# Attention and two MLPs on one core: another order and split of the work for the first tile of tokens

## The chip, the cores and the metric

The kernel runs on one core of one Trainium2 chip. The metric is the device time of one execution in microseconds (us). A core has TensorE for matmuls (PE in the rows; PEld is its weight load), VectorE (DVE), ScalarE (ACT), GpSimd (POOL) and SyncE (SP, here only a queue that issues transfers). SPq and POOLq are the queues' own issuing time.

## The reference, cut to what matters

Chunked attention with 8 batches, 8 heads, 576 tokens and 64 numbers a head, then two feed-forward layers, all in float32.

```
scores = scale * q_c @ k_c.T            # inside chunks of 64 tokens
attn   = exp(scores - max(scores)) ; attn = attn / (sum(attn) + 1e-9)
x      = attn @ v_c                     # 4608 tokens x 512
x      = relu(x @ w_in_a)**2 @ w_out_a  # 512 -> 2048 -> 512
h      = x @ w_in_b
out    = where(h >= 1, h, where(h <= -1, 0, (h + 1)**2 / 4)) @ w_out_b
```

## The kernel before

The 4608 tokens are cut into 9 tiles of 512, a tile into 4 groups of 128 tokens (two chunks, 8 heads). Float32 products of the two MLPs are made of three rounded ones: each matrix is split into a high and a low part, so x, the hidden values and the weights each need a "hi" cast (ScalarE) and a "lo" subtraction (VectorE, or GpSimd for weights).

While the MLP of tile t runs, the attention of tile t+1 is spread over its 16 slices. Each slice has 12 matmuls `up` (L350) and 12 `down` (L385 in the first MLP, L389 in the second). The first tile has no such cover: its four groups run ahead of everything, on a path of their own, and this is the part that the change touches. For group g:

- SyncE loads q and k (`load_qk`, L182, four transfers of 128 KB) and v (`load_v`, L191, two).
- TensorE turns q, then k, by matmuls with the identity (`turn`, L403, 8 matmuls) into two banks of `acc`. VectorE copies them out (`copy_qk`, L669 and twice L673: q, and k's even and odd heads apart, between zeros).
- TensorE makes the scores (`score`, L418, 16 matmuls), for odd groups in a bank of `h_ps`, so that two groups' scores can stand at once.
- VectorE finds each head's maximum and the bias (`find_max`, L679, L683). ScalarE makes the exponentials head by head, 8 instructions that also sum (`exponentials`, L535). VectorE adds 1e-9 and inverts (`invert`, L689, L691), GpSimd multiplies (`normalise`, L281).
- TensorE turns the probabilities (`turn_probs`, L431, 32 matmuls), ScalarE copies them to a block diagonal (`copy_turned`, L547), TensorE multiplies v by it (`head_out`, L449, 16 matmuls). The result is split into x hi (L552, once L779 on VectorE) and x lo (L645).

Then come the first MLP slices f = 0 and 1 of tile 0 in two halves of 256 tokens (`up_half`, L363): the first halves need groups 0 and 1, the second ones all four. Slices 2 to 15 run whole. Group 4 is the first of tile 1; its scores stand between `up_half` and slice 0's `down`, and its q and k are turned by TensorE as well. From group 5 on VectorE turns q and k by 16 block transposes (L660) and the probabilities by 8 (L709), in a fixed order among its `hid_lo` subtractions (L736).

GpSimd loads the weights slice by slice (`load_in` L257, `load_out` L264, 256 KB each) into two places each; ScalarE casts them (L514, L520), GpSimd subtracts (L270, L275). A third load of a kind waits for the first one's subtraction.

Every engine runs its list in the order written; between engines there are only counting semaphores. So the order of the lists, which the change rewrites for the first tile, decides who waits.

## Time and profile before

| | us |
|---|---|
| median of 3 runs | 1685.73 (1684.38 to 1686.45) |
| the profiled execution, its own time | 1684.03 |
| its span | 1682.2 |
| TensorE busy | 1659.6 |
| VectorE, ScalarE, GpSimd busy | 870.6, 623.7, 130.7 |

The span runs from the first to the last instruction of the trace. The profiled execution took 1.8 us more than its span, and 1.7 us less than the median. "Idle before" in a row is time in which the engine had nothing running, with the instruction that ended it behind an arrow. Where the profile holds no clock record yet, at the start, it prints a granted clock of 1.00.

### The profile page before, as it was taken

The page shows a single profiled execution, that of the slowest core. Times are in us where ns is not written, and L with a number is a line of the kernel's source. Part 1 is how long each engine was busy: PE and PEld are TensorE (multiplying, and loading weights), DVE is VectorE, ACT ScalarE, POOL GpSimd, SP SyncE. Part 2 cuts the span into 40 slices and gives each one's busy share as a digit, 9 for nine tenths or more (in the row PEclk, how much of TensorE's full clock was granted, in tenths as well). Part 3 has the DMA queues.
Part 4 walks back from the last instruction along what each step waited for, and adds up shares of the span by engine and source line. Part 5 has one row for each costly group of instructions (what it writes and reads, how often), then busy time and mean ns, then how long its engine had stood idle before and what let it go on. Part 6 is the DMA issues. An engine that isn't in the chain of part 4 may idle for free.

```text
span 1682.2 us, 22443 instructions
## 1 busy us (share of the span) xinstructions
PE 1659.6 (99%) x8256; PEld 1369.8 (81%) x8256; DVE 870.6 (52%) x1630; ACT 623.7 (37%) x1476; POOL 130.7 (8%) x139
## 2 busy tenths in 40 slices
PE   6999999999999999999999999999999999999999
PEld 5788888888888888888888888888888888888887
DVE  4776666666666676674113444443444444344433
ACT  4664444444444444443553222222222222222222
POOL 3650000000000000000472000000000000000000
PEclk9999999999999999999999999999999999999999
DMA  7442111121212121120331010101010101010000
GB/s 157 119 107 64 38 48 35 52 49 26 58 38 63 27 56 39 26 63 26 108 98 70 1 51 1 51 1 52 1 50 1 51 1 50 1 34 17 16 10 26
DMA packets 126670, 74.93 MB, mean 45 GB/s; under 512 B 115552, under 2 KB 115552, under 8 KB 124256
## 3 DMA queue, kind: packets, MB, share of 16 engines
q1 hardware_dynamic: 121440, 56.64, 12.5%
q0 software_dynamic: 5120, 16.78, 3.3%
q8 instruction: 74, 1.21, 0.3%
q14 instruction: 36, 0.29, 0.1%
HBM read 54.53 MB, written 18.87 MB: 44 GB/s over the span
## 4 chain that ended last, share of the span: by engine, by line
PE 97%; DVE 1%; DMA 1%; SPq 0%; issue 0%; ACT 0%
PE h_ps L350 46%; PE acc L385 24%; PE acc L389 23%; PE heads_out_ps L449 2%; PE scores_ps L418 2%; DMA qk_in<-in_k_dram 1%; SPq L182 0%; PE acc L403 0%; PE h_ps L363 0%; DVE q_t_and_k_t_by_head L660 0%; PE acc L431 0%; PE acc L449 0%; DVE hidden_split L736 0%; DVE v_and_probs_diag L709 0%; DVE x_t_split L645 0%
## 5 line engine op out<-in xcount | busy, mean ns | idle before, releaser
L350 PE MATMUL h_ps<-x_t_split,w_in_split 128*128 128x512 f32 x3432 | 825.3, 389 | 1.1 <-issue 1.1
L350 PEld LDWEIGHTS h_ps<-x_t_split,w_in_split 128*128 128x128 f32 x3432 | 644.2, 188 | 136.3 <-issue 3.1
L385 PE MATMUL acc<-hidden_split,w_out_split 128*128 128x512 f32 x1728 | 419.5, 392 | 3.3 <-DVE hidden_split L736 3.3
L389 PE MATMUL acc<-w_out_split,hidden_split 128*128 128x512 f32 x1728 | 415.2, 389 | 0.9 <-DVE hidden_split L736 0.9
L385 PEld LDWEIGHTS acc<-hidden_split,w_out_split 128*128 128x128 f32 x1728 | 321.9, 188 | 74.8 <-issue 9.3
L389 PEld LDWEIGHTS acc<-w_out_split,hidden_split 128*128 128x128 f32 x1728 | 324.2, 188 | 68.5 <-ACT hidden_split L571 1.3
L736 DVE TENSOR_TENSOR hidden_split<-hidden_raw,hidden_split 128x512 fp32r<-128x512 f32 x288 | 199.8, 694 | 317.4 <-ACT hidden_split L571 317.3
L731 DVE SCALAR_TENSOR_TENSOR hidden_raw<-hidden_raw 128x512 f32<-128x512 f32 x144 | 99.7, 692 | 353.0 <-ACT hidden_raw L566 353.0
L571 ACT CAST hidden_split<-hidden_raw 128x512 fp32r<-128x512 f32 x288 | 178.7, 621 | 218.2 <-DVE hidden_raw L734 213.6
L561 ACT ACTIVATE hidden_raw<-h_ps 128x512 f32<-128x512 f32 x144 | 86.1, 598 | 424.6 <-PE h_ps L350 423.1
L566 ACT ACTIVATE hidden_raw<-h_ps 128x512 f32<-128x512 f32 x144 | 86.1, 598 | 369.0 <-PE h_ps L350 369.0
L660 DVE STREAM_TRANSPOSE q_t_and_k_t_by_head<-qk_in 32x256 f32<-32x256 f32 x496 | 216.1, 436 | 8.0
L709 DVE STREAM_TRANSPOSE v_and_probs_diag<-probs 32x256 f32<-32x256 f32 x256 | 111.6, 436 | 3.5
L734 DVE TENSOR_TENSOR hidden_raw<-h_ps,hidden_raw 128x512 f32<-128x512 f32 x144 | 99.5, 691 | 4.9
L563 ACT ACTIVATE hidden_raw<-hidden_raw 128x512 f32<-128x512 f32 x144 | 91.0, 632 | 4.6
L535 ACT ACTIVATE probs<-scores_ps,exp_bias 128x64 f32<-128x64 f32 x272 | 81.0, 324 | 26.0 <-DVE exp_bias L683 26.0
L679 DVE TENSOR_REDUCE score_max<-scores_ps 128x8 f32<-128x512 f32 x34 | 23.5, 691 | 90.0 <-PE scores_ps L418 89.9
L257 POOL DMA_DIRECT2D qk_in<-in_moe_w_in_dram x16 | 12.2, 765 | 655.0 <-DVE q_t_and_k_t_by_head L660 650.8
L535 ACT ACTIVATION_READ_ACCUMULATOR probs<-scores_ps,exp_bias 128x1 f32 x272 | 58.9, 217 | 0.0
L418 PE MATMUL scores_ps<-q_t_and_k_t_by_head 128*64 128x128 f32 x544 | 36.5, 278 | 2.3 <-DVE q_t_and_k_t_by_head L673 2.3
L449 PEld LDWEIGHTS heads_out_ps<-v_and_probs_diag 128*64 128x64 f32 x544 | 29.0, 136 | 11.5 <-issue 11.3
L449 PE MATMUL heads_out_ps<-v_and_probs_diag 128*64 128x128 f32 x544 | 37.2, 279 | 0.0
(60 smaller groups left out, 444.6 us busy)
## 6 DMA issues: line engine op xcount, KB each, us to landing
qk_in<-in_q_dram SPq DMA_DIRECT2D x72, 128.0 KB, 3.0
qk_in<-in_k_dram SPq DMA_DIRECT2D x72, 128.0 KB, 3.1
v_and_probs_diag<-in_v_dram SPq DMA_DIRECT2D x72, 128.0 KB, 3.0
mlp_out_t<-stage SPq DMA_DIRECT2D x9, 1024.0 KB, 4.3
v_and_probs_diag<-mlp_out_t SPq DMA_DIRECT2D x9, 1024.0 KB, 7.0
out_dram<-stage SPq DMA_DIRECT2D x8, 1024.0 KB, 5.0
stage<-in_moe_w_in_dram POOLq DMA_DIRECT2D x16, 256.0 KB, 3.3
stage<-in_moe_w_out_dram POOLq DMA_DIRECT2D x16, 256.0 KB, 3.5
```

Of the source, the lines that this page charges most:

```text
L350: last = nc.tensor.matmul(h_ps[:, bank, :], w_in[:, kt, w, cols], x_t[:, par, x, kt, :], start=(kt == 0 and w == HI and x == HI), stop=(kt ...
L385: last = nc.tensor.matmul(acc[:, j, :], w_out[:, f, w, cols], hid[:, half, x, :], start=first, stop=end)
L389: last = nc.tensor.matmul(acc[:, j, :], hid[:, half, w, cols], w_out[:, f, x, :], start=first, stop=end)
L449: last = nc.tensor.matmul(out_ps_of(n)[rows, head // 2, :], v_in[:, par, head * D:(head + 1) * D], probs_diag_of(n)[:, head, :], start=Tru ...
L535: last = nc.scalar.activation(probs_of(n)[:, pair, keys], s_ps_of(n)[:, pair, keys], ACT.Exp, scale=SCALE, bias=bias[:, par, head:head + 1 ...
L563: nc.scalar.activation(raw[:, half, :], raw[:, half, :], ACT.Square).then_inc(raw_ready, 1)
L571: nc.scalar.copy(hid[:, half, HI, :], raw[:, half, :]).then_inc(hid_hi, 1)
L660: last = nc.vector.transpose(dst, src)
L709: last = nc.vector.transpose(probs_diag[at:at + BLK, :, tok * BLK:(tok + 1) * BLK], heads[tok * BLK:(tok + 1) * BLK, :, wid * BLK:(wid + 1 ...
L731: nc.vector.scalar_tensor_tensor(out=a, in0=a, scalar=1.0, in1=a, op0=ALU.min, op1=ALU.mult).then_inc(squared, 1)
L734: nc.vector.tensor_tensor(a, h_ps[:, half, :], a, ALU.max).then_inc(raw_ready, 1)
L736: nc.vector.tensor_tensor(hid[:, half, LO, :], a, hid[:, half, HI, :].bitcast(F32), ALU.subtract).then_inc(hid_lo, 1)
```

## The change

It rewrites the first tile's path and what goes with it:

- TensorE runs 10 identity matmuls (128x128) into `out_ps` as soon as the identity stands, ahead of the first `turn`.
- k of groups 0 and 1 is loaded from ScalarE's queue (4 transfers), q of both from SyncE's. q and k of group 2 are issued ahead of v of group 0.
- The copies after `turn` are split: ScalarE copies q and k's odd heads, VectorE k's even heads. Group 4's are all made on VectorE.
- Softmax of groups 0 to 3: VectorE takes the maximum, subtracts it for the whole row (PSUM to SBUF), ScalarE makes one exponential of 128x512 in place of 8 of 128x64, VectorE sums by a reduction of its own. Group 3 is normalised on VectorE.
- The scores of all groups stand in one bank; `score(n)` waits until the group before has been shifted.
- GpSimd's first weight load stands behind its first `normalise`, and its order after that is new. ScalarE casts the first input weights after the fourth exponential, the second ones after x hi of group 2 and the turned copy of group 3. TensorE's order at the end of the path is new: `turn(4)` moves behind head_out(1) and turn_probs(2).
- In slice f = 1 of tile 0 VectorE makes `hid_lo` first and normalises and turns group 4 after it.

```diff
@@ SyncE, GpSimd
                     for which, blocks in ((0, q_blocks), (1, k_blocks)):
+                        if which == 1 and not past(g, 2):
+                            continue
...
+            load_qk(2, 0)
             load_v(0, 0)
-            load_qk(2, 0)
...
-            pool.wait_ge(k_turned, 1)
+            normalise(0, 0)
             load_in(0, 0, stage)
-            normalise(0, 0)
+            normalise(1, 1)
             load_in(1, 0, stage)
+            normalise(2, 0)
+            load_out(0, 0, stage)
             weights_in(0, 0, stage)
-            normalise(1, 1)
-            load_out(0, 0, stage)
             load_in(2, 0, stage)
-            normalise(2, 0)
             load_out(1, 0, stage)
             weights_in(1, 0, stage)
-            normalise(3, 1)
@@ TensorE
-                if f == 1:
-                    pe.wait_ge(exped, GROUPS)
...
-                elif n >= 2:
-                    pe.wait_ge(exped, n - 1)
+                elif n > 0:
+                    pe.wait_ge(shifted, n)
...
+            for i in range(WARM):
+                nc.tensor.matmul(out_ps[:, i % HP, :], ident[:], ident[:], start=True, stop=True)
             turn(0)
             for g in range(GROUPS):
                 score(g)
                 if g + 1 < GROUPS:
                     turn(g + 1)
-                else:
-                    turn(GROUPS)
-                if g >= 1:
-                    turn_probs(g - 1)
-                if g >= 2:
-                    head_out(g - 2, g % 2)
-            head_out(GROUPS - 2, 0)
+                    if g >= 1:
+                        turn_probs(g - 1)
+                    if g >= 2:
+                        head_out(g - 2, g % 2)
+            head_out(1, 1)
+            turn_probs(2)
+            turn(GROUPS)
             up_half(0, 0)
-            turn_probs(GROUPS - 1)
+            turn_probs(3)
+            head_out(2, 0)
             up_half(1, 0)
-            head_out(GROUPS - 1, 1)
+            head_out(3, 1)
@@ ScalarE
+            def copy_q(g):
+                act.wait_ge(q_turned, g + 1)
+                if g > 0:
+                    act.wait_ge(scored, g)
+                nc.scalar.copy(qk_t[:, :, 0, :], acc[:, 0, :].rearrange("p (hp n) -> p hp n", hp=HP))
+                act.wait_ge(k_turned, g + 1)
+                if g == 0:
+                    act.wait_ge(k_zero, 1)
+                nc.scalar.copy(qk_t[D:2 * D, :, 2, :], acc[D:2 * D, 1, :].rearrange(
+                    "p (hp n) -> p hp n", hp=HP)).then_inc(q_copied, 1)
+            def exponentiate(n):
+                act.wait_ge(shifted, n + 1)
+                nc.scalar.activation(probs_of(n), probs_of(n), ACT.Exp, scale=SCALE).then_inc(exped, 1)
...
+            for g in range(2):
+                for j in range(2):
+                    c = 2 * g + j
+                    act.dma_start(qk_in[j * CHUNK:(j + 1) * CHUNK, g, 1, :].rearrange("t (h d) -> t h d", d=D),
+                                  k_blocks[c // CPB, c % CPB]).then_inc(qk_loaded[g], DMA)
+            copy_q(0)
+            for g in range(GROUPS):
+                if g + 1 < GROUPS:
+                    copy_q(g + 1)
+                if g == GROUPS - 1:
+                    x_in_hi(0, 0, 0)
+                    x_in_hi(1, 0, 1)
+                exponentiate(g)
+                if g == GROUPS - 1:
                     weights_in(0, 0, stage)
+                if g >= 1:
                     copy_turned(g - 1)
+            x_in_hi(2, 0, 2)
+            copy_turned(3)
+            weights_in(1, 0, stage)
+            x_in_hi(3, 0, 3)
@@ VectorE
+            def shift(n):
+                dve.wait_ge(scored, n + 1)
+                nc.vector.tensor_reduce(top[:], s_ps[:].rearrange(by_head, n=CHUNK), AX.X, ALU.max).then_inc(maxed, 1)
+                dve.wait_ge(maxed, n + 1)
+                if n >= 2:
+                    dve.wait_ge(p_turned, n - 1)
+                nc.vector.tensor_tensor(probs_of(n).rearrange(by_head, n=CHUNK), s_ps[:].rearrange(by_head, n=CHUNK),
+                                        top[:].unsqueeze(2).to_broadcast([P, H, CHUNK]), ALU.subtract).then_inc(shifted, 1)
+            def add_up(n, par):
+                dve.wait_ge(exped, n + 1)
+                if n >= 2:
+                    dve.wait_ge(guarded, n - 1)
+                nc.vector.tensor_reduce(total[:, par, :], probs_of(n).rearrange(by_head, n=CHUNK), AX.X,
+                                        ALU.add).then_inc(summed, 1)
+                dve.wait_ge(summed, n + 1)
...
-                    if attends and (r == 0 and not begins or not past(t, 1) and f == 1):
+                    if attends and r == 0 and not begins:
                         normalise(n, g % 2)
-                    if attends and r in (1, 2):
+                    if attends and r in (1, 2) and not first:
                         turn_probs(n, r - 1)
...
+                    if attends and first:
+                        normalise(n, 0)
+                        turn_probs(n, 0)
...
+            copy_k(0, False)
+            for g in range(GROUPS):
+                shift(g)
+                if g + 1 < GROUPS:
+                    copy_k(g + 1, False)
+                    add_up(g, g % 2)
                     invert(g, g % 2)
+            x_in_lo(0, 0, 0)
+            add_up(3, 1)
+            normalise(3, 1)
+            x_in_lo(1, 0, 1)
+            copy_k(GROUPS, True)
+            x_in_lo(2, 0, 2)
+            x_in_lo(3, 0, 3)
```

## Rows read from the trace of the kernel before

**Rows 1.** Stretches: from:to, length, TensorE busy (instructions), granted clock, DMA share, GB/s.

```profile
26.50:30.00 3.50, 3.50 (x47) 0.53 0.27 76
...
49.33:52.20 2.87, 0.00 (x0) 1.00 0.09 34
52.20:1682.00 1629.80, 1624.70 (x7872) 1.00 0.15 41
```

**Rows 2.** The chain that ended last, in time: start us, us, what held it.

```profile
2.87 3.45 DMA qk_in<-in_k_dram
...
6.46 1.96 PE acc L403 x8
...
9.88 1.98 PE scores_ps L418 x16
...
19.59 6.49 DMA qk_in<-in_k_dram
...
26.13 1.45 PE acc L403 x8
27.58 1.91 PE acc L431 x32
29.49 1.28 PE acc L449 x16
...
32.26 1.70 PE h_ps L363 x12
...
35.04 1.62 PE h_ps L363 x12
36.67 1.05 PE acc L449 x16
...
37.74 0.59 ACT x_t_split L552
...
38.35 0.70 DVE x_t_split L645
...
51.12 0.97 DVE hidden_split L736
```

**Rows 3.** Busy time of five engines, granted clock, DMA share and GB/s, first loads.

```profile
2.50:6.50 4.00, 0.04 (x1) 0.07 (x2) 0.52 (x1) 0.00 (x0) 0.00 (x0) 1.00 0.84 187
```

**Rows 4.** The timeline, 0 to 60 us: start, us, engine, line, operation, shapes, idle before.

```profile
0.75 1.28 ACT L535 ACT_TABLE_LOAD   x1 [0.75 <-PEq L812]
...
8.44 1.39 DVE L673 COPY q_t_and_k_t_by_head<-acc 64x512 f32<-64x512 f32 x2
...
15.55 0.20 DVE L691 RECIPROCAL prob_sum_inverse<-prob_sum_inverse 128x8 f32<-128x8 f32 x1
...
16.13 0.69 DVE L679 TENSOR_REDUCE score_max<-h_ps 128x8 f32<-128x512 f32 x1 [0.38 <-PE h_ps L418]
...
20.00 1.09 PE L403 MATMUL acc<-ident,qk_in 128*128 128x128 f32 x8
...
23.07 1.09 PE L418 MATMUL h_ps<-q_t_and_k_t_by_head 128*64 128x128 f32 x16
...
30.73 0.62 ACT L514 CAST w_in_split<-stage 128x512 fp32r<-128x512 f32 x1
...
31.44 1.26 POOL L270 TENSOR_TENSOR w_in_split<-stage,w_in_split 128x512 fp32r<-128x512 f32 x1 [5.71 <-ACT w_in_split L514]
...
33.89 1.15 PE L431 MATMUL acc<-ident,probs_spare 128*64 128x64 f32 x32
...
35.09 1.17 ACT L547 COPY hidden_raw<-acc 64x512 f32<-64x512 f32 x2 [3.74 <-PE acc L431]
...
44.57 3.57 DVE L660 STREAM_TRANSPOSE q_t_and_k_t_by_head<-qk_in 32x256 f32<-32x256 f32 x8
...
49.05 0.62 ACT L571 CAST hidden_split<-hidden_raw 128x512 fp32r<-128x512 f32 x1
...
56.69 1.79 DVE L660 STREAM_TRANSPOSE q_t_and_k_t_by_head<-qk_in 32x256 f32<-32x256 f32 x4
```

More of the change, by code:

```diff
@@ L40 @@
 TURNS = (0, 3, 8, 12, 16)
+WARM = 10
 def past(count, n):
@@ L398, in turn @@
                 if g > 0:
-                    pe.wait_ge(qk_copied, g)
+                    pe.wait_ge(q_copied, g)
+                    pe.wait_ge(k_copied, g)
                 for which, turned in ((0, q_turned), (1, k_turned)):
@@ L417, in score @@
                         rows = slice(c * CHUNK, (c + 1) * CHUNK)
-                        last = nc.tensor.matmul(s_ps_of(n)[rows, hp, :], qk_t[:, hp, 0, rows], qk_t[:, hp, 1:3, rows],
+                        last = nc.tensor.matmul(s_ps[rows, hp, :], qk_t[:, hp, 0, rows], qk_t[:, hp, 1:3, rows],
                                                 start=True, stop=True)
@@ L604, in split_x @@
                 nc.scalar.copy(x_t[:, 1 - par, HI, kt, :], x_in[:, kt, :]).then_inc(x_hi, 1)
-            for g in range(GROUPS + 2):
-                if g < GROUPS:
-                    exponentials(g, g % 2)
-                if g == 0:
+            for g in range(2):
[12 more added lines that the diff above has]
+                if g == GROUPS - 1:
                     weights_in(0, 0, stage)
-                if 1 <= g <= GROUPS:
+                if g >= 1:
                     copy_turned(g - 1)
-                if g == GROUPS - 1:
-                    weights_in(1, 0, stage)
-                if g >= 2 and g != 3:
-                    x_in_hi(g - 2, 0, g - 2)
+            x_in_hi(2, 0, 2)
+            copy_turned(3)
+            weights_in(1, 0, stage)
+            x_in_hi(3, 0, 3)
             for f in range(2):
@@ L662, in turn, with copy_k @@
                     last.then_inc(qk_turned, 1)
-            def copy_qk(g):
-                dve.wait_ge(q_turned, g + 1)
+            def copy_k(g, all_of_it):
+                dve.wait_ge(k_turned, g + 1)
                 if g > 0:
                     dve.wait_ge(scored, g)
-                nc.vector.tensor_copy(qk_t[:, :, 0, :], acc[:, 0, :].rearrange("p (hp n) -> p hp n", hp=HP))
-                dve.wait_ge(k_turned, g + 1)
-                for head in range(2):
-                    rows = slice(head * D, (head + 1) * D)
-                    last = nc.vector.tensor_copy(qk_t[rows, :, 1 + head, :], acc[rows, 1, :].rearrange(
-                        "p (hp n) -> p hp n", hp=HP))
-                last.then_inc(qk_copied, 1)
+                nc.vector.tensor_copy(qk_t[0:D, :, 1, :], acc[0:D, 1, :].rearrange(
+                    "p (hp n) -> p hp n", hp=HP)).then_inc(k_copied, 1)
+                if all_of_it:
+                    nc.vector.tensor_copy(qk_t[:, :, 0, :], acc[:, 0, :].rearrange("p (hp n) -> p hp n", hp=HP))
+                    nc.vector.tensor_copy(qk_t[D:2 * D, :, 2, :], acc[D:2 * D, 1, :].rearrange(
+                        "p (hp n) -> p hp n", hp=HP)).then_inc(q_copied, 1)
@@ L680, in find_max @@
                 dve.wait_ge(maxed, n + 1)
-                if past(n, 2):
+                if past(n, EARLY):
                     dve.wait_ge(exped, n - 1)
@@ L693, in normalise @@
             def normalise(n, par):
-                heads = probs[:].rearrange(by_head, n=CHUNK)
+                heads = probs_of(n).rearrange(by_head, n=CHUNK)
                 invert(n, par)
                 dve.wait_ge(inverted, n + 1)
+                if not past(n, GROUPS):
+                    dve.wait_ge(normed, n)
                 nc.vector.tensor_tensor(heads, heads, inv[:, par, :].unsqueeze(2).to_broadcast([P, H, CHUNK]),
@@ L720, in tile @@
                     begins = not past(t, 1) and f == 0
-                    if attends and (r == 0 and not begins or not past(t, 1) and f == 1):
+                    first = not past(t, 1) and f == 1
+                    if attends and r == 0 and not begins:
                         normalise(n, g % 2)
-                    if attends and r in (1, 2):
+                    if attends and r in (1, 2) and not first:
                         turn_probs(n, r - 1)
@@ L765, in _ @@
             dve.wait_ge(k_zero, 1)
-            copy_qk(0)
-            for g in range(GROUPS + 3):
-                if g < GROUPS:
-                    find_max(g, g % 2)
-                    copy_qk(g + 1)
-                if g >= 3 and g != 4:
-                    x_in_lo(g - 3, 0, g - 3)
-                if g < GROUPS:
-                    invert(g, g % 2)
-                if g == 3:
-                    dve.wait_ge(headed, 2)
-                    nc.vector.tensor_copy(x_t[:, 0, HI, :, GROUP:2 * GROUP], out_ps_of(1)).then_inc(x_hi, 1)
-                    x_in_lo(1, 0, 1)
+            copy_k(0, False)
[4 more added lines that the diff above has]
+                    add_up(g, g % 2)
+                    invert(g, g % 2)
+            x_in_lo(0, 0, 0)
[5 more added lines that the diff above has]
+            x_in_lo(3, 0, 3)
             tile(0, 0, 0, True)
```

23 lines of the change are left out of this document (10 added, 13 removed).

## The prediction

> **What bounds the kernel now.** I read the stretches first, then the chain of waits, then the timeline of the first 60 us. From 52.2 us to 1682 TensorE is busy 1624.70 of 1629.80 us at full clock [rows 1], on matmuls that the change doesn't touch. So the change can only move the moment from which TensorE runs without a pause. I follow four of its marks: score(3) at 23.07 [rows 4], the first up_half at 32.26, the second at 35.0 [rows 2], and the end of VectorE's sixteen block transposes of group 5, 56.69 + 1.79 = 58.48 [rows 4], on which score(5) waits. In the chain [rows 2] the reader sees four kinds of link there: loads (2.87 to 6.32, 19.59 to 26.08), TensorE's own work, copies and casts, and once VectorE's order (hid_lo of slice 1, at 51.12). The clock is part of it. Eight identity matmuls take 1.96 us at 6.46 and 1.09 at 20.00 [rows 2, 4]. 16 score matmuls take 1.98 at 9.88 and 1.09 at 23.07. [...] It fell again after the pause from 24.16 to 26.13: 0.53 from 26.5 to 30 [rows 1].
>
> **Step 1, loads and first scores.** Before, q and k of group 0 were issued one after another, the last at 2.87, landed 3.45 later [rows 2]. On two queues the last issue is at about 1.5: landing at 4.97 if issuing were all, 6.32 if the transfer engines were. From 2.5 to 6.5 they were busy 0.84 at 187 GB/s [rows 3], so two queues can add a fifth at most; I take 6.0. [...]
> Turning q and k: 1.96 at the slow clock, to 8.0. Copies: before, two of VectorE's 0.70 still to do when k was turned (1.39 [rows 4]), now one beside ScalarE's. Score(0) starts at 8.75 instead of 9.88. The ten identity matmuls run from 1.5 on, 1.96 / 8 = 0.245 each, so 2.5 us: done by 4.0, hidden by the load. At full clock turn and score would win 0.87 + 0.89. I leave these out of the sum (a pause of 2 us follows the ten) and keep them for the range.
>
> **Step 2, the group loop.** Score(0) ends at 10.7; maximum and subtraction are 2 x 0.71 on VectorE (0.69 [rows 4] and a gap), the copy of k 0.71: score(1) at 12.9. ScalarE has meanwhile copied for group 1, 1.2 us from 11.3 to 12.5. What follows there is the table load, 1.28 [rows 4]: in the kernel before it ran at 0.75, under the first load, since the exponential was ScalarE's first work. Now copies stand ahead of it, and the load goes with the exponential. So the exponential (0.65, as a cast of this size [rows 4]) ends at 14.45. VectorE waits for it, then 0.71 for the sum, 0.45 for the two small ones (0.20 [rows 4] each, and gaps), then maximum, subtraction and copy of the next group, 2.13: score(2) at 17.8. Bounds of the table load: 1.28 won back if it isn't there, 1.28 lost in step 1 if it stands ahead of the k transfers.
> From there TensorE is the longest: score, turn, turn_probs, head_out are 1.09 + 1.09 + 1.15 + 1.05 = 4.38 [rows 2, 4], some 4.25 where neighbours overlap, against VectorE's 4 x 0.71 + 0.45 = 3.3. Score(3) comes at 22.1, 1.0 earlier than before. That exponentials are 8 x 0.3 us shorter buys nothing more, as they lay beside VectorE's copies.
>
> **Step 3, to the first up_half.** The load of q and k 4 ended TensorE's wait at 26.13 [rows 2]; now turn(4) stands two blocks later, and that stall goes. Next late is x lo of group 1. Score(3) and head_out(1) end at 24.2, x hi 24.8, the exponential 25.5, then on VectorE sum, small ones, normalise, x lo: 0.71 + 0.45 + 0.71 + 0.71 = 2.6: 28.1. TensorE ends turn_probs(2) and turn(4) at 26.4 and waits 1.7. The weight split is there in time: cast 0.62 and subtraction 1.26 [rows 4] from 25.5 on, 27.5. First up_half at 28.15, 4.1 earlier.
>
> **Step 4, the second up_half.** This gives it all back. up_half 1.62, turn_probs(3) 1.10, head_out(2) 1.05: 31.9. up_half(1, 0) needs the second input weights split. Before, ScalarE cast them at 30.73 and GpSimd was done at 32.70 [rows 4]. Now the cast stands behind x hi of group 2 and the turned copy of group 3, and x hi of group 2 waits for that very head_out(2). Behind 31.9: 0.62 for x hi, 1.20 for the copies (1.17 [rows 4]), 0.65 for the cast, 1.30 for GpSimd, gaps 0.15: 35.85. TensorE stands for 3.9 us, with head_out(3) queued behind the waiting matmul. Against 35.0: **+0.9**. The rest to the last two up_halves (36.67, 37.74, 38.35 [rows 2]) is as before.
>
> **Step 5, the clock.** The pause of 2.0 us before 26.13 was followed by a slow stretch, in which blocks took 1.45, 1.91 and 1.28 (four, 32 and 16 matmuls' work that takes 1.09, 1.15, 1.05 at full clock): 1.35 lost, all on the chain [rows 2, 4]. The pause of 2.87 before 52.2 was not [rows 1]. One of 3.9 us most likely is. Behind it stand up_half (1.62) and head_out (1.05), which would take up to twice that, 2.7 more; the last two up_halves another 3.2 at the worst. Bounds 0 and 5.9; since the old slow stretch was over by 30 (1.28 at 29.49 is nearly full speed again) [rows 1, 2], I take 1.8: **+1.8**.
>
> **Step 6, slices 0 to 2.** Before, VectorE had work without a gap from 44.57 to 58.48 [rows 4]: transposes of group 5 until 48.14, normalise and transposes of group 4, hid_lo of slice 1 at 51.12, the rest. Now hid_lo comes first, and waits for ScalarE's cast, 49.05 + 0.62 = 49.67 [rows 4]: VectorE stands from 48.14 to 49.7, 1.55 us, with normalise and all transposes queued behind. down(1) starts 1.7 earlier, but the transposes end later, and head_out(4) and score(5) wait for them. The cost is 1.55 less what the two hid_lo lose no more to company (0.97 and as much against 0.70): 1.0 to 1.55. I take **+1.3**. The low bound is 0, if the weights on which ScalarE waits land sooner.
>
> **Sum.** 0.9 + 1.8 + 1.3 = 4.0 us. The profiled execution took 1684.03, 1.7 below the median; such a one would take 1688.0, and the median 1685.73 + 4.0 = **1689.7**, slower by 0.24%. I call 0.2% (3.4 us) about what a measurement can tell.
>
> **Rivals.**
> - *The clock takes the change's side* (ends as no change). The ten matmuls make the engine fast by the first data, or soon after, and the pause of step 4 is not punished. Then step 1 gives up to 0.87 + 0.89 and step 5 falls: 4.0 - 1.75 - 1.8 = +0.4, 1686.2. For it: 4 us of nearly gapless work came before the fast stretch. Against it: the pause is twice the one that was punished. It decides from the point where no slow block follows head_out(2).
> - *The table load is elsewhere* and hidden. -1.3 from step 2, which carries through to head_out(2): +2.7, 1688.4. For it: a copy may need the table too, so that it would load behind the transfers and under the first wait. [...]
> - *The slow clock lasts* through the last two up_halves: +3.2 more, 1692.9.
> - *Faster*: the second weights are in time. That takes x hi of group 2 early, so head_out(2) ahead by the whole 3.9 us, which needs first scores at the 4.97 bound, the fast clock and no table load at once; or a cost of cast and GpSimd far under the rows'. With no stall step 4 turns to -3.0, step 5 to 0, together -1.7; with the fast clock in step 1 -3.5, 1682.2.
>
> **How the numbers follow.** The forecast 0.44, of which a sixth falls under 3.4 us; clock on the change's side 0.18; table load elsewhere 0.12; slow clock lasts 0.09; faster 0.17. Slower 0.46, same 0.37, faster 0.17. The range leaves a tenth on either side: 1682.8, near the last rival, to 1693.2, the third. The likeliest case's own range is 1688.2 to 1691.5 (steps 5 and 6 by their bounds, less the extremes).
>
> **What would show it.** Right: the load of group 0 landing near 6.0; a table load of 1.28 between copies and exponential at 12.5; score(3) near 22; first up_half near 28; TensorE idle 3 to 4 us before the second up_half, released by GpSimd's subtraction; then blocks at half speed; VectorE idle before hid_lo of slice 1; a wait before head_out(4) or score(5). Wrong: a second up_half before 34 (steps 1, 2 or 4), the blocks behind it at 1.62 and 1.05 (step 5), or transposes of group 5 that end less than 15 us after down(0) starts (step 6).

## The result and the profile after

The changed kernel is slower by 0.30%: 1691.12 us against 1685.99, medians of ten runs each, ratio 1.0030 (95% interval 1.0017 to 1.0044). That is 5.1 us more, where 4.0 were forecast. The profiled execution took 1687.67 us, with a span of 1685.9; it is among the quicker of the ten.

The ten runs spread over 8.8 us, those of the kernel before over 3.2. Each run's record has the mean granted clock of TensorE, and the two go together:

```
us     1686.45 1687.67 1688.35 1688.92 1690.27 1691.98 1693.18 1693.34 1694.58 1695.23
clock  0.998   0.997   0.997   0.997   0.996   0.995   0.994   0.994   0.993   0.993
```

From 0.998 to 0.993 the run grows by 8.8 us, 1.76 for each thousandth. A thousandth of the mean is 3.4 us spent at half speed (0.50, as in the stretches below) instead of full, in which 1.7 us of work is lost: an estimate from the span of 1685.9. (The clock is given to a thousandth, so 1.76 is good to a fifth or so.) So nearly the whole spread can be put down to the time for which the clock was low, and the median of 1691.12 contains more of it than the profiled 1687.67.

**TensorE in the profile after.** The timeline of the first 66 us, PE's lines; the columns are those of [rows 4].

```profile
1.54 4.64 PE L473 MATMUL heads_out_ps<-ident 128*128 128x128 f32 x20 [1.54 <-POOL ident L287]
6.22 1.53 PE L401 MATMUL acc<-ident,qk_in 128*128 128x128 f32 x8
8.69 1.09 PE L417 MATMUL scores_ps<-q_t_and_k_t_by_head 128*64 128x128 f32 x16 [0.94 <-DVE q_t_and_k_t_by_head L696]
...
18.07 1.09 PE L401 MATMUL acc<-ident,qk_in 128*128 128x128 f32 x8 [1.46 <-DMA qk_in<-in_k_dram]
...
20.95 1.04 PE L417 MATMUL scores_ps<-q_t_and_k_t_by_head 128*64 128x128 f32 x16
...
26.17 1.09 PE L401 MATMUL acc<-ident,qk_in 128*128 128x128 f32 x8 [2.08 <-DMA qk_in<-in_k_dram]
27.62 2.93 PE L360 MATMUL h_ps<-x_t_split,w_in_split 128*128 128x256 f32 x12 [0.36 <-DVE x_t_split L672]
30.48 1.40 PE L430 MATMUL acc<-ident,probs_spare 128*64 128x64 f32 x32
...
36.58 1.85 PE L360 MATMUL h_ps<-x_t_split,w_in_split 128*128 128x256 f32 x12 [3.82 <-POOL w_in_split L271]
38.37 1.98 PE L448 MATMUL acc<-hidden_raw,v_and_probs_diag 128*64 128x128 f32 x16
41.75 4.42 PE L360 MATMUL h_ps<-x_t_split,w_in_split 128*128 128x256 f32 x24 [1.41 <-DVE x_t_split L672]
...
47.50 2.98 PE L382 MATMUL acc<-hidden_split,w_out_split 128*128 128x512 f32 x12 [0.31 <-DVE hidden_split L784]
...
61.21 1.09 PE L448 MATMUL heads_out_ps<-v_and_probs_diag 128*64 128x128 f32 x16 [1.80 <-DVE v_and_probs_diag L756]
64.12 1.09 PE L417 MATMUL scores_ps<-q_t_and_k_t_by_head 128*64 128x128 f32 x16 [1.82 <-DVE q_t_and_k_t_by_head L687]
```

The kernel before has these marks behind [rows 4], in the same view (down(0), score(5) and down(2)):

```profile
43.61 3.00 PE L385 MATMUL acc<-hidden_split,w_out_split 128*128 128x512 f32 x12 [0.36 <-DVE hidden_split L736]
...
58.81 1.04 PE L418 MATMUL scores_ps<-q_t_and_k_t_by_head 128*64 128x128 f32 x16
59.78 3.01 PE L385 MATMUL acc<-hidden_split,w_out_split 128*128 128x512 f32 x12
```

Read the marks one after another, before to after: score(3) 23.07 to 20.95; the first up_half 32.26 to 27.62, 4.6 us won; the second up_half 34.97 (35.04 in the chain of [rows 2]) to 36.58, all of it gone and 1.6 more; down(0) 43.61 to 47.50, 3.9 behind; score(5) 58.81 to 64.12, 5.3 behind. From down(2) to the end the profile before needs 1682.2 - 59.78 = 1622.4 us, and the profile after 1685.9 - 65.15 = 1620.75; in twelve further kernels this rest took 1620.6 to 1623.1. So in these profiles the difference is made ahead of down(2), as the prediction assumed. What lies behind it differs by a microsecond or two from execution to execution.

**The clock** of stretches of the profile after (columns of [rows 1], with the busy time of the other engines in between):

```profile
28.00:30.00 2.00, 2.00 (x11) 2.00 (x11) 1.45 (x3) 0.00 (x0) 0.00 (x0) 0.50 1.12 244
34.00:36.00 2.00, 0.00 (x0) 0.00 (x0) 0.11 (x1) 1.07 (x2) 0.82 (x1) 1.00 0.58 131
38.00:40.00 2.00, 2.00 (x19) 1.72 (x17) 0.00 (x0) 0.00 (x0) 0.00 (x0) 0.50 0.41 139
42.00:44.00 2.00, 2.00 (x10) 2.00 (x11) 0.00 (x0) 0.01 (x1) 1.68 (x3) 0.50 0.78 176
```

The engine had stood 2.08 us before 26.17 and 3.82 before 36.58. Behind each pause it came to run at 0.50, though not at once: turn(4) at 26.17 still took 1.09, and the up_half at 36.58 took 1.85, with a mean of 0.86 from 36.5 to 38.4. The slow blocks are the ones behind these: 12 matmuls in 2.93 instead of 1.70, 16 in 1.98 instead of 1.09, 24 in 4.42 instead of 3.13.

**ScalarE, VectorE and GpSimd**, from the same timeline:

```profile
0.75 3.05 ACTq L627 DMA_DIRECT2D qk_in<-in_k_dram  x4
3.83 1.28 ACT L544 ACT_TABLE_LOAD   x1 [3.83 <-issue]
```
```profile
21.35 0.17 DVE L734 TENSOR_SCALAR prob_sum_inverse<-prob_sum 128x8 f32<-128x8 f32 x1
...
24.88 1.13 DVE L734 TENSOR_SCALAR prob_sum_inverse<-prob_sum 128x8 f32<-128x8 f32 x1
...
52.89 0.69 DVE L784 TENSOR_TENSOR hidden_split<-hidden_raw,hidden_split 128x512 fp32r<-128x512 f32 x1 [0.86 <-ACT hidden_split L588]
53.49 1.28 DVE L734 TENSOR_SCALAR prob_sum_inverse<-prob_sum 128x8 f32<-128x8 f32 x1
```
```profile
24.72 1.25 POOL L271 TENSOR_TENSOR w_in_split<-stage,w_in_split 128x512 fp32r<-128x512 f32 x1 [1.30 <-ACT w_in_split L517]
...
53.46 1.28 POOL L271 TENSOR_TENSOR w_in_split<-stage,w_in_split 128x512 fp32r<-128x512 f32 x1 [1.71 <-ACT w_in_split L517]
```

The table load stands at 3.83, right behind ScalarE's four transfers and ahead of its first copy (7.35), under the wait for the first data. VectorE's small addition, 0.17 us when alone, took 1.13 and 1.28 when GpSimd was in a subtraction: the first ended at 26.01, GpSimd's at 25.97, and the second at 54.77, GpSimd's at 54.74. Why it takes so long the trace doesn't say; g4_gpsimd_apart tries whether it takes 0.17 with GpSimd out of the way.

### The profile page after: what moved, and what is told of

Its sections match the earlier page's. It is cut to its first block, busy times and chain, and to the rows that moved or that the text cites. A ratio compares the mean times of both kernels' runs of the same rounds, so it can differ in the third digit from the quotient of the medians.

```text
span 1685.9 us, 22430 instructions
## 1 busy us (share of the span) xinstructions
PE 1663.6 (99%) x8276; PEld 1374.4 (82%) x8276; DVE 870.1 (52%) x1626; ACT 621.8 (37%) x1425; POOL 129.6 (8%) x138
## 3 DMA queue, kind: packets, MB, share of 16 engines
q1 hardware_dynamic: 119328, 56.11, 12.5%
## 4 chain that ended last, share of the span: by engine, by line
PE 97%; DVE 1%; ACT 1%; DMA 1%; SPq 0%; issue 0%; POOL 0%
PE h_ps L349 46%; PE acc L382 23%; PE acc L386 23%; PE heads_out_ps L448 2%; PE scores_ps L417 2%; PE h_ps L360 0%; SPq L183 0%; DMA qk_in<-in_q_dram 0%; DMA qk_in<-in_k_dram 0%; DVE q_t_and_k_t_by_head L687 0%; DVE v_and_probs_diag L756 0%; PE acc L448 0%; PE acc L401 0%; DVE hidden_split L784 0%; ACT probs L535 0%
## 5 line engine op out<-in xcount | busy, mean ns | idle before, releaser
L535 ACT ACTIVATE probs<-scores_ps,exp_bias 128x64 f32<-128x64 f32 x256 | 76.2, 324 | 17.6 <-DVE exp_bias L728 17.6
L724 DVE TENSOR_REDUCE score_max<-scores_ps 128x8 f32<-128x512 f32 x32 | 22.1, 691 | 87.6 <-PE scores_ps L417 87.6
L535 ACT ACTIVATION_READ_ACCUMULATOR probs<-scores_ps,exp_bias 128x1 f32 x256 | 55.4, 216 | 0.0
```

The costliest lines, as they stand in the source:

```text
L535: last = nc.scalar.activation(probs_of(n)[:, pair, keys], s_ps[:, pair, keys], ACT.Exp, scale=SCALE, bias=bias[:, par, head:head + 1], acc ...
```

## The experiments

Twelve further kernels in three groups (e, f and g), each group on a chip of its own beside runs of the kernel before (medians 1686.43, 1686.08 and 1686.45, which the ratios are against). The ratio is worked out from all runs together and not from the two medians: for e3_both the medians differ by 2.6 us and the ratio says 3.9, for g3_before_warm 4.2 and 5.4. Marks and spans are of each kernel's profiled execution, which may lie anywhere in its runs' spread. "Up 2" is the second up_half, "n" the number of runs.

| kernel | score(3) | up 2 | down(0) | down(2) | span | median (lowest to highest), n | ratio [95%] |
|---|---|---|---|---|---|---|---|
| after | 20.95 | 36.58 | 47.50 | 65.15 | 1685.9 | 1691.12 (1686.45 to 1695.23), 10 | 1.0030 [1.0017, 1.0044] |
| e1_cast_early | 21.73 | 31.98 | 40.82 | 60.24 | 1681.6 | 1685.67 (1681.89 to 1687.57), 11 | 0.9992 [0.9983, 1.0001] |
| e2_slice1_order | 19.80 | 35.80 | 45.66 | 63.13 | 1683.9 | 1687.48 (1683.09 to 1693.84), 9 | 1.0008 [0.9993, 1.0023] |
| e3_both | 24.49 | 36.68 | 45.53 | 61.41 | 1682.0 | 1683.80 (1680.08 to 1685.01), 7 | 0.9977 [0.9966, 0.9989] |
| e4_fill_pause | 19.95 | 35.07 | 43.69 | 62.42 | 1685.5 | 1687.18 (1685.17 to 1689.91), 11 | 1.0006 [0.9997, 1.0015] |
| f1_no_warm | 23.29 | 35.08 | 43.94 | 62.90 | 1685.1 | 1684.97 (1682.63 to 1688.36), 11 | 0.9992 [0.9983, 1.0001] |
| f2_one_queue | 20.28 | 30.93 | 39.77 | 57.40 | 1678.7 | 1681.25 (1677.77 to 1686.34), 12 | 0.9973 [0.9963, 0.9983] |
| f3_turn4_late | 21.41 | 34.00 | 42.64 | 60.13 | 1681.4 | 1684.21 (1680.04 to 1685.95), 11 | 0.9984 [0.9976, 0.9993] |
| f5_qk3_first | 19.67 | 33.14 | 41.98 | 59.49 | 1680.7 | 1681.68 (1679.86 to 1685.49), 10 | 0.9977 [0.9968, 0.9986] |
| g1_one_queue_qk3 | 20.18 | 32.32 | 41.16 | 57.02 | 1678.1 | 1680.59 (1679.90 to 1682.98), 5 | 0.9965 [0.9952, 0.9979] |
| g2_filled | 19.55 | 30.58 | 39.42 | 55.35 | 1676.2 | 1679.49 (1678.03 to 1680.13), 5 | 0.9955 [0.9941, 0.9969] |
| g3_before_warm | 21.36 | 33.16 | 41.81 | 60.80 | 1681.8 | 1682.22 (1679.14 to 1683.57), 7 | 0.9968 [0.9956, 0.9979] |
| g4_gpsimd_apart | 20.64 | 30.74 | 39.58 | 55.43 | 1676.0 | 1680.82 (1677.81 to 1683.16), 6 | 0.9966 [0.9954, 0.9978] |

### The two places that the prediction names

**The cast of the second weights, ahead of what it stood behind** (e1_cast_early, ScalarE):

```diff
                     copy_turned(g - 1)
+            weights_in(1, 0, stage)
             x_in_hi(2, 0, 2)
             copy_turned(3)
-            weights_in(1, 0, stage)
```

> The changed kernel, with ScalarE's cast of the second input weights moved ahead of x hi of group 2 and the turned copy of group 3; nothing else. Theory (the late cast makes TensorE stand 3.8 us before the second up_half, and the slow clock behind it costs some 3 more): that pause falls under 1 us, the blocks behind it run at full speed, and the kernel gains 4 to 6 us on the changed one, which puts it at 1685 to 1687, level with the kernel before. Rival (the loss is made elsewhere, in slices 0 to 2 or in the groups; the pause only shifts it): the pause goes and another takes its place, gain under 1.5 us.

The median went from 1691.12 to 1685.67, 5.4 us down. The prediction had priced just this ("with no stall"): a sum of -1.7 in place of +4.0, 5.7 less. PE's timeline:

```profile
31.98 1.70 PE L360 MATMUL h_ps<-x_t_split,w_in_split 128*128 128x256 f32 x12
33.80 1.09 PE L448 MATMUL acc<-hidden_raw,v_and_probs_diag 128*64 128x128 f32 x16
36.31 3.13 PE L360 MATMUL h_ps<-x_t_split,w_in_split 128*128 128x256 f32 x24 [1.41 <-DVE x_t_split L672]
```

No idle time stands before the second up_half, and the blocks behind it run at full clock (1.00 from 31.98 to 39.40). In this profile down(0) is 6.7 us ahead of the changed kernel's. Not all of it lasts: down(2) is 4.9 ahead and the span 4.3 shorter, as TensorE waits 1.39 us before down(1), where it was 0.52, and the clock falls behind the waits of 1.76 and 1.82 before head_out(4) and score(5) (0.50 from 58.34 to 60.3; score(5) takes 1.98, down(2) 3.55).

**VectorE's order in slice 1 as before** (normalise and transposes of group 4 ahead of hid_lo; e2_slice1_order):

```diff
-                    if attends and r == 0 and not begins:
+                    if attends and (r == 0 and not begins or first):
                         normalise(n, g % 2)
-                    if attends and r in (1, 2) and not first:
+                    if attends and r in (1, 2):
                         turn_probs(n, r - 1)
...
-                    if attends and first:
-                        normalise(n, 0)
-                        turn_probs(n, 0)
```

> The changed kernel, with VectorE's order in slice 1 of tile 0 as before (normalise and turned probabilities of group 4 ahead of hid lo). Theory: down(1) starts some 1.5 us later, but head_out(4) and score(5) start 0.8 to 1.7 us earlier, and the kernel gains about 1.3 us (1.0 to 1.7) on the changed one. Rival (hid lo first is what lets down(1) start, and its gain holds): down(2) starts later and the kernel loses 1 to 1.5 us.

3.6 us less than the changed kernel in the median, more than the 1.0 to 1.7 expected. The intervals of the two ratios overlap, so the sign is likely and the size isn't known. Its timeline shows what the old order costs in its turn:

```profile
54.00 4.56 PE L382 MATMUL acc<-hidden_split,w_out_split 128*128 128x512 f32 x12 [2.64 <-DVE hidden_split L784]
...
61.24 1.09 PE L448 MATMUL heads_out_ps<-v_and_probs_diag 128*64 128x128 f32 x16
62.16 1.04 PE L417 MATMUL scores_ps<-q_t_and_k_t_by_head 128*64 128x128 f32 x16
```

The waits before head_out(4) and score(5) are gone. But TensorE now stands 2.64 us before down(1), and here the clock fell behind that pause (0.63 from 54.0 to 58.5): 4.56 instead of 3.0. From down(0) to score(5) it is 16.5 us, of which 1.6 is the slow clock; without it 14.9, against 15.2 before and 16.6 after.

**Both** (e3_both, the two edits together; from here on "the mended kernel"):

> Both edits of the two runs beside it. Theory: the gains add, 5 to 7 us on the changed kernel, 1684 to 1686, which is 0 to 2 us under the kernel before. Rival (both remove the same wait): no more than the larger of the two.

1683.80, 2.6 us faster than the kernel before (0.9977) and 7.3 faster than the changed one. The prediction's terms give -1.7 without step 4's stall, and -3.0 without step 6 as well. The single gains of 5.4 and 3.6 would add to 9.0; whether they fall short of adding, the runs can't tell.

**Matmuls in the pause**, which stays (e4_fill_pause, 14 identity matmuls into a bank of scores that is free then):

```diff
             head_out(2, 0)
+            for i in range(14):
+                nc.tensor.matmul(s_ps[:, i % HP, :], ident[:], ident[:], start=True, stop=True)
             up_half(1, 0)
```

> The changed kernel with 14 more identity matmuls (results unused) between head_out(2) and the second up_half, inside the pause of 3.8 us, 14 x 0.23 = 3.2 us of work at full clock. The wait for the second weights stays. Theory (part of the loss is the clock behind the pause): the second up_half starts where it did, near 36.6 or a little later, but it and head_out(3) and the two last up_halves take 1.7, 1.1 and 3.1 us, and the median gains 1.5 to 3 us. Rival (the clock falls whatever is done, or costs nothing on the path): no gain, or up to 0.7 us lost where the work runs past the pause.

```profile
31.16 3.39 PE L490 MATMUL scores_ps<-ident 128*128 128x128 f32 x28
35.07 1.67 PE L360 MATMUL h_ps<-x_t_split,w_in_split 128*128 128x256 f32 x12 [0.51 <-POOL w_in_split L271]
36.66 1.09 PE L448 MATMUL acc<-hidden_raw,v_and_probs_diag 128*64 128x128 f32 x16
```

The useless work took 3.39 of what had been idle; up_half still waits for GpSimd, but runs in 1.67 and head_out in 1.09, at a granted clock of 1.00. The median is 3.9 us lower than the changed kernel's, and the spread 4.7 us instead of 8.8. The intervals (up to 1.0015 here, from 1.0017 there) just miss each other. So the slow clock behind that pause is worth some 3.9 us by itself, more than the 1.5 to 3 expected. It can't simply be taken from the 5.4 of the early cast, as if the pause of 3.8 us cost only the other 1.5: e1 closes the pause too, and gives some of it back in the slices, as its profile shows. The second up_half comes 1.5 us sooner here than in the changed kernel only because this execution was that much ahead already (head_out(2) at 30.19, there 31.71).

### From the mended kernel, one part each

**Without the ten matmuls** (f1_no_warm, `WARM = 0`):

> The version with both orders mended (cast early, slice 1 as before: 1683.8 us), without the ten identity matmuls ahead of the first data. Theory (they make the engine fast by the first data, so turn(0), score(0) and turn(1) run in 1.1 us each and not in 2.0, 2.0 and 1.7): first score some 0.5 us later, score(1) some 2 us later, of which the wait for q and k of group 3 (2.3 to 2.7 us of pause before turn(3)) swallows most; loss 0 to 1.5 us. Rival (all of the first blocks' time is on the path): loss 2 to 3 us.

1684.97 against 1683.80, a loss of 1.2 us, within the 0 to 1.5 expected, with intervals that overlap. The early blocks are back at the slow clock:

```profile
6.44 1.94 PE L401 MATMUL acc<-ident,qk_in 128*128 128x128 f32 x8 [6.44 <-DMA qk_in<-in_q_dram]
9.32 1.98 PE L417 MATMUL scores_ps<-q_t_and_k_t_by_head 128*64 128x128 f32 x16 [0.94 <-DVE q_t_and_k_t_by_head L696]
```

Turning takes 1.94 and not 1.09, scores 1.98 and not 1.09. What is left of the change without the ten is not to be told from the kernel before (0.9992, 0.9983 to 1.0001).

**k of groups 0 and 1 back on SyncE's queue** (f2_one_queue):

```diff
-                        if which == 1 and not past(g, 2):
-                            continue
...
-            for g in range(2):
-                for j in range(2):
-                    c = 2 * g + j
-                    act.dma_start(qk_in[...], k_blocks[c // CPB, c % CPB]).then_inc(qk_loaded[g], DMA)
```

> The same mended version, with k of groups 0 and 1 issued from SyncE's queue again, after q of the same half group. Theory (the transfer engines limit, so the second queue saves some 0.1 to 0.4 us of landing): group 0 lands at 6.3 and not at 6.2, but the later issues on SyncE's queue start up to 1.3 us later, which meets the wait for group 3; loss 0 to 1 us. Rival (the second queue is worth its saved issue time of 1.35 us on the path): turn(0) starts 1.3 us later, loss 1.3 us or more.

The first `turn` of the mended kernel and then of this one:

```profile
6.51 1.09 PE L401 MATMUL acc<-ident,qk_in 128*128 128x128 f32 x8 [0.88 <-DMA qk_in<-in_q_dram]
```
```profile
6.56 1.09 PE L399 MATMUL acc<-ident,qk_in 128*128 128x128 f32 x8 [0.83 <-DMA qk_in<-in_k_dram]
```

The first data come 0.05 us sooner on two queues, which is nothing: over the profiles `turn(0)` starts between 6.22 and 6.66 on two queues and between 6.18 and 6.56 on one. From 2.5 to 6.5 us the transfers moved 209 GB/s on two queues and 187 on one, in these two profiles. Nor do later loads gain: the loads of group 2 wait for `turn(0)` and are issued from 7.78 on in the changed kernel, from 7.69 on here. The median is even 2.5 us lower with one queue, which neither expectation had, but the intervals overlap.

**turn(4) behind head_out(2)** (f3_turn4_late), its copies behind x lo of group 2:

```diff
-            turn(GROUPS)
             up_half(0, 0)
...
             head_out(2, 0)
+            turn(GROUPS)
             up_half(1, 0)
@@ VectorE
-            copy_k(GROUPS, True)
             x_in_lo(2, 0, 2)
+            copy_k(GROUPS, True)
```

> The same mended version, with turn(4) behind head_out(2) and VectorE's copies of it behind x lo of group 2. Theory (turn(4) was hidden under the wait for x lo of group 1 in most executions, so only the pause grows): no change within 0.8 us. Rival (turn(4)'s wait for its load sets the first up_half, or its absence there lengthens the pause so that the clock falls more often): 1 us faster in the one case, 1 to 2 us slower in the other.

```profile
28.08 2.55 PE L360 MATMUL h_ps<-x_t_split,w_in_split 128*128 128x256 f32 x12 [3.54 <-DVE x_t_split L672]
```

No gain, as expected: 1684.21 against 1683.80. The wait for the load of group 4 was only taken over: TensorE now stands 3.54 us in one piece for x lo of group 1, and the first up_half is slow behind it.

**q and k of group 3 ahead of v of group 0** (f5_qk3_first) in SyncE's queue:

```diff
             load_qk(2, 0)
-            load_v(0, 0)
             load_qk(3, 1)
+            load_v(0, 0)
```

> The same mended version, with the loads of q and k of group 3 issued ahead of v of group 0. Theory (after the change the group loop is bound by the loads: turn(3) waits 2.3 to 2.7 us for q and k of group 3): group 3's issue starts 1.3 us earlier, turn(3) too, the pause before it falls to 1.3 us and less often slows the clock; gain 1 to 2.5 us on 1683.8. Rival (the transfer engines are full whatever the order, or the loop is bound elsewhere): turn(3) starts where it did, or the wait moves to v of group 0 or to the next block; gain under 0.5 us.

```profile
16.40 1.10 PE L401 MATMUL acc<-ident,qk_in 128*128 128x128 f32 x8
...
22.67 1.09 PE L448 MATMUL acc<-hidden_raw,v_and_probs_diag 128*64 128x128 f32 x16 [1.95 <-DMA v_and_probs_diag<-in_v_dram]
```

turn(3) no longer waits (18.07 in the changed kernel, 19.12 in the mended one's profile), but the wait moves to v of group 1, 1.95 us before head_out(1), as the rival said. The median is 1681.68, 2.1 below the mended kernel, which is the theory's size, with intervals that overlap.

### The best version, and what the ten matmuls are worth alone

**One queue and q, k of group 3 first** (g1_one_queue_qk3, the edits of f2_one_queue and f5_qk3_first together):

> The mended version with both: k of groups 0 and 1 on SyncE's queue again (1681.3 us alone) and q and k of group 3 ahead of v of group 0 (1681.7 us alone). Theory (both shorten the wait of turn(3) for group 3's load, 2.65 us in the mended version, to 0.88 and 0): their gains overlap, 1679.5 to 1681.5. Rival (the one-queue version's gain has another source, such as transfers of later groups that meet less traffic): they add, 1678 to 1679.5. If two queues had been worth something, this version would be slower than 1681.7.

1680.59 (0.9965) in five runs with a spread of 3.1 us, inside the theory's 1679.5 to 1681.5. One pause is left in the slices:

```profile
49.51 2.97 PE L380 MATMUL acc<-hidden_split,w_out_split 128*128 128x512 f32 x12 [2.64 <-DVE hidden_split L777]
```

**Matmuls in that pause too** (g2_filled):

```diff
+                    if not past(t, 1) and f == 2:
+                        for i in range(9):
+                            nc.tensor.matmul(out_ps[:, i % HP, :], ident[:], ident[:], start=True, stop=True)
                     if f > 0:
```

> The version of the run beside it, with nine identity matmuls (results unused, 9 x 0.23 = 2.1 us at full clock) between up(2) and down(1), where TensorE stands 2.6 to 2.9 us for hid lo of slice 1. Theory (the pause itself is VectorE's and stays, the slow clock that followed it in the profiled executions of four versions, where down(1) took 4.2 to 5.5 us and not 3.0, goes): down(1) starts where it did and takes 3.0 us, gain 0.7 to 2 us on the version beside it. Rival (no gain, since the slow stretch is then drawn by another pause, or the matmuls push down(1) back): within 0.5 us.

```profile
45.00 2.17 PE L463 MATMUL heads_out_ps<-ident 128*128 128x128 f32 x18
47.80 3.00 PE L380 MATMUL acc<-hidden_split,w_out_split 128*128 128x512 f32 x12 [0.64 <-DVE hidden_split L780]
```

1679.49, 7.0 us below the kernel before (0.9955, 0.9941 to 0.9969) and below both kernels of the case. The mean granted clock is 0.999 or 1.000 in all five runs, and they spread over 2.1 us. Against the version without the nine matmuls it is 1.1 us, with intervals that overlap, so what the nine add isn't shown.

**The kernel before with the ten matmuls alone** (g3_before_warm):

```diff
             pe.wait_ge(ident_ready, 1)
+            for i in range(10):
+                nc.tensor.matmul(out_ps[:, i % HP, :], ident[:], ident[:], start=True, stop=True)
             turn(0)
```

> The kernel before, with the ten identity matmuls ahead of turn(0) and nothing else of the change. Theory (they bring full clock to turn(0), score(0) and turn(1)): the first scores end 1.7 to 2.3 us earlier, but the pause before 26.13, which the load of q and k of group 4 ends, takes most of it; 0 to 1.5 us faster than before. Rival (worth its full 2 us or more): 2 to 2.6 us faster.

1682.22, 4.2 us faster (0.9968): more than either expectation. Its timeline:

```profile
6.34 1.09 PE L403 MATMUL acc<-ident,qk_in 128*128 128x128 f32 x8 [0.60 <-DMA qk_in<-in_k_dram]
...
21.36 1.09 PE L418 MATMUL h_ps<-q_t_and_k_t_by_head 128*64 128x128 f32 x16
24.38 1.10 PE L403 MATMUL acc<-ident,qk_in 128*128 128x128 f32 x8 [1.93 <-DMA qk_in<-in_k_dram]
...
50.57 5.46 PE L385 MATMUL acc<-hidden_split,w_out_split 128*128 128x512 f32 x12 [3.06 <-DVE hidden_split L738]
```

Score(3) comes at 21.36 and not 23.07. The wait for the load of group 4 keeps its length (1.93, before 1.96) but moves forward with it, to 24.38 from 26.13, and down(0) starts at 41.81, 1.8 earlier. So the landing of that load is no fixed date. Only 1.8 of the 4.2 us are seen there. The profiled execution doesn't help with the rest, as it is the slowest of the seven: down(1) lost 2.5 to the clock.

**GpSimd's first weight split held back until VectorE's normalise of group 3** (g4_gpsimd_apart, `pool.wait_ge(normed, GROUPS)` ahead of `weights_in(0)`):

> The mended version (two queues, group order of the change), with GpSimd's first weight subtraction held until VectorE has normalised group 3. Theory (VectorE's small instruction of 0.17 us took 1.13 to 1.14 because it ran into GpSimd's subtraction of 1.25): that instruction takes 0.17 to 0.3, x lo of group 1 comes 0.9 us earlier, but the weights then come 0.5 us after it, so the first up_half gains 0.3 to 0.5 us and the median at most 0.6. Rival (the small instruction is long for another reason, such as its wait): it stays at 1.1 and the first up_half comes 1 us later.

VectorE, GpSimd and TensorE in its timeline:

```profile
24.57 0.17 DVE L735 TENSOR_SCALAR prob_sum_inverse<-prob_sum 128x8 f32<-128x8 f32 x1
...
25.79 1.26 POOL L271 TENSOR_TENSOR w_in_split<-stage,w_in_split 128x512 fp32r<-128x512 f32 x1 [2.68 <-DVE probs_spare L745]
...
27.20 1.66 PE L361 MATMUL h_ps<-x_t_split,w_in_split 128*128 128x256 f32 x12 [0.60 <-POOL w_in_split L271]
```

With GpSimd out of the way the same instruction takes 0.17: the collision is shown. But the first up_half now waits for GpSimd instead, so that from that group's maximum to up_half it is 5.47 us, and in the changed kernel 5.58: 0.1 won. The median is 1680.82, 3.0 below the mended kernel; the intervals overlap, and 0.1 us does not explain it.

## Why the prediction was right, and where its steps were not

Slower by 0.24% was forecast and 0.30% measured (0.17% to 0.44%); the time of 1691.12 lies 1.4 us above 1689.7, inside the likeliest case's own range. The mechanism is the one forecast: the late cast, the slow clock behind the pause, VectorE's new order. That the size came out so close is in part luck, as the steps show:

**Step 1** was mis-sized. Group 0 landed at 6.18, forecast 6.0. But the ten matmuls took 4.64 us, not 2.5, and stand in the trace as x20 (L473). The price had been taken from `turn`'s transpositions of the same size, whose eight calls stand as x8 (1.96 us). That a matmul call can stand as two instructions could have been read from the rows of before, where score's eight calls (L418) stand as x16. So hardly a pause followed them (6.18 to 6.22), by the blocks' times the clock rose during `turn(0)` (1.53, then 1.09 for score(0)), and the part that I had left out of the sum was there: score(0) at 8.69 in 1.09 us, where 8.75 in 1.98 was forecast. In other profiles, again by the times, the clock rose within the ten (3.95 us in g2) and stayed up over a pause of up to 1.14 us (f3, turn(0) in 1.09). The first half of the rival "the clock takes the change's side" came true.

**Step 2** was wrong about the table load, and the rival was right: it ran at 3.83, hidden. That it goes with the exponential was my assumption, from its line in before (L535, ScalarE's first work there), and no run shows it: the trace lists the load under the line of ScalarE's first copy (L544), at 3.83, where the first exponential ran at 11.61. In f2, where ScalarE issues no transfers, it stands at 0.75 under that same copy's line (L542 there), 6.5 us ahead of the copy. In the sum of step 2 the 1.28 us at 12.5 had no counterpart in the trace. With both gains score(3) would have come at 22.1 - 0.9 - 1.3 = 19.9. It came at 20.95, since turn(3) waited 1.46 us for q and k of group 3, a load that I hadn't followed. f5, g1 and g2 show that wait to be one of SyncE's order: with group 3 first it is gone in all three. And its length is chance. Seven of the profiled kernels have the same instructions up to turn(3), and it waited 0.54 us (e2), 0.74 (e4), 1.41 (g4), 1.46 (after), 1.91 (f3), 2.25 (e1) and 2.65 (e3), with score(3) at 19.80 in the first and at 24.49 in the last, where the clock fell too. So the marks of two profiles can differ by some 2 us, and with the clock by over 4, without any cause in the kernels.

**Step 3** forecast 28.15 and got 27.62, but by errors that nearly cancel: 1.15 more was won before score(3), and 1.0 was lost to the collision at 24.88; the rest are smaller terms. That the stall for the load of group 4 goes was wrong: turn(4) stood 2.08 us for it. It was hidden, as VectorE was late anyway (0.36 still to wait behind it), but the clock fell behind it (0.51 from 27.6 to 30.5): 2.93 + 1.40 for what costs 1.70 + 1.15, 1.5 us that the sum had at nothing.

**Step 4** was right: idle time of 3.82 forecast as 3.9, released by GpSimd's subtraction, at 36.58 against 35.85 forecast. The 0.7 come from ahead of the pause: head_out(2) ended at 32.8 where 31.9 was forecast (1.5 of slow clock less an up_half 0.5 sooner), and the chain behind it took 3.8 and not 3.95. e1 shows the cause, and that the stall with its clock is worth 5.4 us of median.

**Step 5** was right in its mechanism, with 1.8 for it. In the profile the blocks behind the second pause lost 0.15 + 0.89 + 1.29 = 2.3. Over the runs it is more: e4, which fills that pause and changes nothing else, is 3.9 us below in the median, twice the term and within its bounds of 0 to 5.9. (A slip of reading: the block of 1.45 us that the term was judged by is `turn(4)`, eight matmuls and not four.) The rival "the slow clock lasts", through the last two up_halves, is what the profile shows in part (4.42 against 3.13); the median of 1691.12 lies about halfway between the forecast and that rival's 1692.9.

**Step 6** was right in size and not in its parts: 16.62 against 15.20 from down(0) to score(5), 1.4 for 1.3 forecast. VectorE stood only 0.86 us, since the cast came sooner after the transposes; another 1.1 was the collision with GpSimd at 53.49. e2 shows the order to be the cause. The runs also show what the sum left out, the clock on both sides. The new order shortens the wait before down(1) (2.90 to 0.52 us), and the old one's pause there costs the clock in some executions (4.2 to 5.5 us for 3.0 in the profiles of e2, f1, f2, f3, f5 and g3). But the new order's two waits of 1.8 us cost it too: score(5) and down(2) took 1.98 + 3.55 in e1 and 1.98 + 4.72 in e4, for 1.09 + 3.0.

**The sum.** By the marks it was 2.7 + 1.3 to score(5); the profile shows 3.9 + 1.4 = 5.3, of which 1.6 isn't in the spans' difference of 3.7. What the sum left out cancels in good part, which is luck: on the side of the gains 0.9 of clock (step 1) and 1.3 of table load (step 2), on the side of the losses 1.0 at score(3) for turn(3)'s wait, 1.0 of collision and 1.5 of clock behind turn(4) (step 3). With a shorter wait for group 3 and no slow clock behind turn(4) this profile would have been some 2.5 us shorter, an estimate from these numbers. The prediction's own arithmetic for the mended kernel (-3.0) agrees with e3 (-2.6), and that for the stall alone (5.7) with e1 (5.4); how the 5.7 divide does not, as e4 puts the clock at 3.9 and not at 1.8.

**What the good parts are worth.** The ten matmuls alone on the old kernel: -4.2. All of the change, mended: -2.6. The intervals of these two overlap. The mended change without them: -1.1 (against 1686.08), not separated from nothing. So the whole-row softmax, the split copies and the second queue have no gain here that these runs can tell from zero.

**Open.** Why the ten matmuls win 4.2 us when 1.8 is seen in the marks; why f2 and g4 have medians 2.5 and 3.0 below the mended kernel's, when their edits win nothing and 0.1 directly. The mean granted clock doesn't tell g3 (0.998 in five of seven runs) from the kernel before (0.998 or 0.999 in eleven of twelve). One thing that bears on the other two was seen: the mended kernel's own profile waited 2.65 us before turn(3), and ran at the slow clock from there to score(3) (0.50 from 19.1 to 24.0); its seven runs fall near 1680 (clock 0.999) or near 1684 (0.996 or 0.997). How often a kernel falls into such a stretch may be what differs, but no run isolates it.

```profile
19.12 1.97 PE L401 MATMUL acc<-ident,qk_in 128*128 128x128 f32 x8 [2.65 <-DMA qk_in<-in_k_dram]
```

## What to carry to other kernels

When a rewrite pulls a path forward, look for the operation that was moved behind something new on another engine: here one cast, two steps later in ScalarE's list, used up a lead of 4.6 us, and moved forward again it won 5.4 in the median. Before two profiles are compared mark by mark, see how much a mark moves between executions with the same instructions (here score(3) from 19.80 to 24.49). Count a pause of TensorE twice, once as time and once as what the slow clock behind it may take (here 3.8 us of pause, and 3.9 of median when e4 filled it), and let useless matmuls run in a pause that can't be closed. Try the cheapest part of a large change by itself before crediting the whole with its gain.

## What the runs showed of the hardware that was not expected

- The identity matmuls and score's stood here as two instructions a call in the trace, `turn`'s transpositions as one: the ten calls as x20 (L473), e4's 14 as x28, g2's nine as x18 and score's eight as x16, but `turn`'s eight of 128x128 as x8 (L401). The x20 took 4.64 us ahead of the first data (0.23 each); the x28 took 3.39 and the x18 2.17, where the profiles show a granted clock of 1.00, 0.12 each.
- Pauses alike in length weren't punished alike. Behind 2.08 us (after, turn(4)) the first up_half took 2.93 us at a granted clock of 0.51, and behind 2.64 us (e2) down(1) took 4.56 at 0.63. Behind 2.47 us (f2) turn(4) and the first up_half took 1.09 and 1.70, and behind 2.64 us (g1) down(1) took 2.97, all at 1.00. The changed kernel, with several such pauses, spread over 8.8 us in ten runs; g2, with two places filled, over 2.1 in five.
- An addition of 128x8 numbers on VectorE took 0.17 us alone, and 1.13 and 1.28 beside a subtraction on GpSimd; both times it ended 0.03 to 0.04 us after GpSimd's. The profile of before has a small VectorE instruction (L683, 0.17 us at 12.63) that did the same: 1.20 us at 60.63, ended at 61.83, where GpSimd subtracts from 60.52 to 61.80.
